# A linear-attention and two-expert-layer kernel: unit 1 directly behind unit 0, two tiles before unit 2, and another order in the first experts and at the pass ends

## The reference, cut

```python
# attention: B, H, S, D = 4, 8, 768, 48, all float32
mag = sqrt(a_re**2 + a_im**2); scale = minimum(mag, 0.999) / (mag + 1e-6)
for t in range(S):
    S_re, S_im = ar*S_re - ai*S_im + outer(k[t], v[t]), ar*S_im + ai*S_re
    y[t] = q[t] @ S_re
# first layer: x (3072 x 384), w_in (384 x 2048), w_out (2048 x 384)
h = x @ w_in
g = where(h >= 1, h, where(h <= -1, 0, (h + 1)**2 / 4))
x = g @ w_out
# second layer: 8 experts, w1 (384 x 1024), w2 (1024 x 384) each
P = exp(logits - max); 8 times: rows of P to 1, columns of P to 1, P *= N / E
out = sum over e of P[:, e] * (maximum(x @ w1[e], 0) @ w2[e])
```

## Time and profile before

| | |
|---|---|
| runs, us | 2284.01, 2279.48, 2281.38 (median 2281.38) |
| profiled execution | 2283.22 us, its span 2281.4 us |
| TensorE busy | 2235.4 us (98%) |
| VectorE, ScalarE, GpSimd busy | 76%, 44%, 21% |
| mean granted TensorE clock | 0.994 of 2.4 GHz |
| instructions | 38084 |

### The profile page before, as it was taken

One profiled execution on the slowest core, in us unless ns is written; L12 is line 12 of the kernel. 1 busy time (PEld: TensorE's weight loads), 2 busy tenths in 40 slices (PEclk: granted clock), 3 DMA queues, 4 the chain that ended last, 5 costly groups with the idle time before them and its releaser, 6 DMA issues. The chain is left out here.

```text
span 2281.4 us, 38084 instructions
## 1 busy us (share of the span) xinstructions
PE 2235.4 (98%) x13741; PEld 2081.1 (91%) x13741; DVE 1728.4 (76%) x3042; ACT 1012.3 (44%) x1716; POOL 467.8 (21%) x310
## 2 busy tenths in 40 slices
PE   5899999999999999999999999999999999999999
PEld 4799999999999889999998999999998999999998
DVE  7788888888855877776778777777777777777775
ACT  6566666566555433344334433344333433334332
POOL 0000000000000423232223322233222322233222
PEclk9899999999999999999999999999999999999999
DMA  5111111111103031111110231111110211101111
GB/s 169 39 52 53 50 50 50 50 50 50 43 29 139 28 111 56 35 49 56 55 56 28 83 111 56 46 37 55 55 55 28 84 56 56 54 30 56 55 56 28
DMA packets 70726, 131.34 MB, mean 58 GB/s; under 512 B 5512, under 2 KB 36488, under 8 KB 70536
## 3 DMA queue, kind: packets, MB, share of 16 engines
q1 hardware_dynamic: 70536, 129.14, 17.4%
HBM read 114.96 MB, written 14.16 MB: 57 GB/s over the span
## 5 line engine op out<-in xcount | busy, mean ns | idle before, releaser
L606 POOL TENSOR_TENSOR h_l<-u_s,h_h 128x512 fp32r<-128x512 f32 x192 | 246.4, 1304 | 1601.5 <-ACT h_h L863 1601.5
L1777 PE MATMUL bank<-w_h,h_h 128*128 128x384 f32 x1536 | 515.7, 336 | 5.0 <-POOL h_l L606 3.8
L1779 PE MATMUL bank<-w_h,h_l 128*128 128x384 f32 x1536 | 514.8, 335 | 0.0
L1778 PE MATMUL bank<-w_l,h_h 128*128 128x384 f32 x1536 | 514.6, 335 | 0.0
L1584 PE MATMUL bank<-x_l,w_h 128*128 128x512 f32 x1056 | 414.6, 393 | 0.0
L1583 PE MATMUL bank<-x_h,w_h 128*128 128x512 f32 x1056 | 414.4, 392 | 0.0
L1585 PE MATMUL bank<-x_h,w_l 128*128 128x512 f32 x1056 | 413.5, 392 | 0.0
L1381 DVE SCALAR_TENSOR_TENSOR acc<-bank,prob,acc 128x384 f32<-128x384 f32 x352 | 214.6, 613 | 183.7 <-PE bank L1779 181.0
L1777 PEld LDWEIGHTS bank<-w_h,h_h 128*128 128x128 f32 x1536 | 289.1, 188 | 9.0 <-POOL h_l L606 5.4
L1778 PEld LDWEIGHTS bank<-w_l,h_h 128*128 128x128 f32 x1536 | 289.0, 188 | 2.0
L852 ACT ACTIVATE p_s<-bank 128x512 f32<-128x512 f32 x96 | 57.4, 598 | 523.2 <-PE bank L1585 522.9
(11 more groups left out here) (188 smaller groups left out, 3999.1 us busy)
## 6 DMA issues: line engine op xcount, KB each, us to landing
stage<-w_ SPq DMA_DIRECT2D x48, 768.0 KB, 6.6
w_raw<-w_ SPq DMA_DIRECT2D x96, 384.0 KB, 3.6
qb<-q_in_ SPq DMA_DIRECT2D x24, 192.0 KB
kb<-k_in_ SPq DMA_DIRECT2D x24, 192.0 KB
vb<-v_in_ SPq DMA_DIRECT2D x24, 192.0 KB
x_hi<-x2h_s SPq DMA_DIRECT2D x36, 128.0 KB, 1.8
x_lo<-x2l_s SPq DMA_DIRECT2D x36, 128.0 KB, 1.8
x_h<-x_hi SPq DMA_DIRECT2D x3, 1536.0 KB, 11.3
```

What stands on the lines that cost most here:

```text
L606: pool.tensor_tensor(tiles_of(h_l, name), group_sum(name), tiles_of(h_h, name).bitcast(F32), ALU.subtract).then_inc(hl_done, 1)
L1777: pe.matmul(dst, h_h[:, f, t_], w2h[:, fw], start=n == 0, stop=False)
L1778: pe.matmul(dst, h_h[:, f, t_], w2l[:, fw], start=False, stop=False)
L1779: mm = pe.matmul(dst, h_l[:, f, t_], w2h[:, fw], start=False, stop=n == 3)
```

## The change

On TensorE units 0 and 1 have a sequence of their own (`first_units`), in which p and r of unit 1 follow x of unit 0, one weight piece goes between r and the products of q and k, and `mm_in(0)`, `mm_in(1)`, `mm_out(0)` follow unit 1. ScalarE and VectorE get matching orders. Units 2 and 3 take tiles from tables. Eight pieces go ahead of the first p, with high parts one more ahead, and twelve pieces' low parts are TensorE's, four VectorE's. `scale_factor` is cut in two, and scale_sum(1) goes between its halves. In group 1 of the experts, `w1_sums` goes ahead of sum 11, `w1_hi` behind the high part of 21_0, and two parts of `w1_lo` ahead of the low part of 22_1; `sink_rows(5)` is no longer cut. Steps 4 and 5 of `xt_sums` go into the loop over y.

```diff
-        LEAD, BY_PE = 7, 13
-        SPLIT_AT = [LEAD + 2, LEAD + 2, LEAD + 4, BY_PE, BY_PE + 1, BY_PE + 2, BY_PE + 3, BY_PE + 3, BY_PE + 3]
+        LEAD, BY_PE = 8, 12
+        SPLIT_AT = {2: ((BY_PE, BY_PE + 2), (BY_PE + 2, BY_PE + 3)), 3: ((BY_PE + 3, 2 * TILES), (0, 0))}
+        def tile_of(u, s_):
+            return {2: (2, None, 3, 4), 3: (5, None, 6, 7)}[u][s_] if u < 4 else 4 * (u - 2) + s_
+        def tile_before(u, s_):
+            return {2: (1, 2, None, 3), 3: (4, 5, None, 6)}[u][s_] if u < 4 else 4 * (u - 2) + s_ - 1
+        def out_of(u, s_):
+            return {2: (None, 1, 2, 3), 3: (None, 4, 5, None)}[u][s_] if u < 4 else 4 * (u - 2) + s_ - 2
...
@@ GpSimd, group @@
                 for name in LOW:
+                    if one and name == "22_1":
+                        w1_lo(g + 1, 1 - j, range(2))
                     h_lo(g, name)
...
-                        w1_lo(g + 1, 1 - j)
+                        w1_lo(g + 1, 1 - j, range(2, 3) if one else range(3))
...
@@ ScalarE @@
+            def first_unit():
+                stacks(0, 0)
+                stacks(0, 1)
+                p_sq(1)
+                p_root(1)
+                first_lo(LEAD + 1, LEAD + 2)
+                scale_sq(3)
+                y_out(0)
+                x_hi(0)
+                scale_root(3)
+                first_hi(LEAD + 3, BY_PE)
+            def second_unit():
+                first_lo(LEAD + 2, LEAD + 3)
+                stacks(1, 0)
+                stacks(1, 1)
+                first_lo(LEAD + 3, BY_PE)
+                scale_sq(4)
+                y_out(1)
+                x_hi(1)
+                g_sq(0)
+                g_hi(0)
+                g_sq(1)
+                p_sq(2)
+                p_root(2)
+                scale_root(4)
...
-            first_hi(0, 1)
+            first_hi(0, 2)
             for i in range(LEAD):
-                first_hi(i + 1, i + 2)
+                first_hi(i + 2, i + 3)
                 first_lo(i, i + 1)
-            first_hi(LEAD + 1, LEAD + 2)
+            first_hi(LEAD + 2, LEAD + 3)
...
                 h_hi(g, "21_0")
+                if one:
+                    for part in range(3):
+                        w1_hi(ex + j, g + 1, 1 - j, part)
...
@@ VectorE, first_unit and second_unit @@
                 scale_sum(3)
-                scale(3)
                 state_add(0)
                 x_lo(0)
...
                 by_k(1)
-                blocks(1, 1, 5)
+                scale(3)
+                blocks(1, 1, 2)
                 masked(1)
-                blocks(1, 5, NI)
+                blocks(1, 2, NI)
+                state_add(1)
                 scan_init(1)
-                scan(1, 0, 2)
-                state_add(1)
-                scan(1, 2, 3)
                 x_lo(1)
+                scan(1, 0, 3)
+                g_max(0)
                 scan(1, 3, 4)
+                g_lo(0)
                 final(2)
...
-            FIRST_LO = {2: ((), (), (), (BY_PE, BY_PE + 1)), 3: ((), (BY_PE + 1, BY_PE + 2), (), ()),
-                        4: ((BY_PE + 2, BY_PE + 3), (), (), ())}
+            FIRST_LO = {2: ((), (), (BY_PE, BY_PE + 2), ()), 3: ((), (), (BY_PE + 2, BY_PE + 3), ()),
+                        4: ((BY_PE + 3, BY_PE + 4), (), (), ())}
...
             scale_sum(0)
+            scale_first(0)
+            scale_sum(1)
             scale_factor(0)
-            scale_sum(1)
             scale_by(0)
...
@@ VectorE, group @@
                 if second:
                     sink_columns(3)
+                    w1_sums(ex + j, g + 1, 1 - j)
...
-                next_x2(4)
+                if j:
+                    next_x2(4)
...
-                next_x2(5)
...
-                if second:
-                    sink_rows(5, (0,))
                 for k in range(PB):
                     if second and k == 2:
-                        sink_rows(5, (1,))
-                    if k == (2 if second else 0) and (nxt or j == 0):
+                        sink_rows(5)
+                    if not second and k == 0 and (nxt or j == 0):
                         w1_sums(ex + j, g + 1, 1 - j)
+                    if j == 0 and k in (5, 6):
+                        next_x2(k - 1)
...
@@ TensorE @@
+            def first_units():
+                first_lo(0, LEAD)
+                p_by_tokens(0)
+                first_lo(LEAD, LEAD + 1)
+                r_by_tokens(0)
+                q_and_k(0)
+                scores(0)
+                first_lo(LEAD + 1, LEAD + 2)
+                y_sum(0)
+                state_sum(0)
+                x_by_channels(0)
+                p_by_tokens(1)
+                r_by_tokens(1)
+                first_lo(LEAD + 2, LEAD + 3)
+                q_and_k(1)
+                scores(1)
+                first_lo(LEAD + 3, BY_PE)
+                y_sum(1)
+                state_sum(1)
+                x_by_channels(1)
+                mm_in(0)
+                mm_in(1)
+                mm_out(0)
...
+            for u in range(2, UNITS):
                 p_by_tokens(u)
+                tile_in(tile_of(u, 0))
                 r_by_tokens(u)
+                tile_out(out_of(u, 0))
                 q_and_k(u)
+                tile_in(tile_of(u, 1))
+                tile_out(out_of(u, 1))
                 scores(u)
+                tile_in(tile_of(u, 2))
+                tile_out(out_of(u, 2))
                 y_sum(u)
                 state_sum(u)
+                tile_in(tile_of(u, 3))
                 x_by_channels(u)
+                tile_out(out_of(u, 3))
```

More of the change, by code:

```diff
@@ L593, in w2_lo, with w1_lo @@
                                        ALU.subtract).then_inc(w2_low, 1)
-            def w1_lo(g, j):
+            def w1_lo(g, j, parts=range(3)):
                 raw_ = quad(j)
                 h, l, to = w1s[j]
-                for part, (w, r_) in enumerate(((slice(W_11, W_22), raw_[:, :, :, 0]),
-                                                (slice(W_22, S_1), raw_[:, 1:3, :, 1]),
-                                                (slice(S_1, NW), to[:, S_1:NW]))):
+                for part in parts:
+                    w, r_ = ((slice(W_11, W_22), raw_[:, :, :, 0]), (slice(W_22, S_1), raw_[:, 1:3, :, 1]),
+                             (slice(S_1, NW), to[:, S_1:NW]))[part]
                     pool.wait_ge(w1_high, g * 3 + part + 1)
@@ L610, in group @@
                 g = ex * QUADS + j
+                one = isinstance(g, int) and g == 1
                 for name in LOW:
+                    if one and name == "22_1":
+                        w1_lo(g + 1, 1 - j, range(2))
                     h_lo(g, name)
@@ L745, in unit @@
                     p_sq(u + 1)
-                tile_hi(t)
-                tile_sq(t + 1)
+                tile_hi(tile_before(u, 1))
+                tile_sq(tile_of(u, 1))
                 if even and u >= 4:
@@ L801, in _ @@
             scale_root(2)
-            for u in range(UNITS):
+            first_unit()
+            second_unit()
+            for u in range(2, UNITS):
                 unit(u)
@@ L874, in group @@
                 g = ex * QUADS + j
-                zero = isinstance(g, int) and g == 0
+                zero, one = (isinstance(g, int) and g == i for i in range(2))
                 keep_p1(g, 0)
@@ L903, in group @@
                 elif nxt or j == 0:
-                    for part in range(3):
-                        w1_hi(ex + j, g + 1, 1 - j, part)
+                    if not one:
+                        for part in range(3):
+                            w1_hi(ex + j, g + 1, 1 - j, part)
                     w2_hi(ex + j, g + 1, 1 - j)
@@ L932, in scale, with scale_first @@
             def scale(u):
+                scale_first(u)
                 scale_factor(u)
                 scale_by(u)
-            def scale_factor(u):
+            def scale_first(u):
                 n = 4 * u
@@ L943, in scale_factor @@
                 dve.scalar_tensor_tensor(yr_u[:], sq[:, 1], 3.0, yr_u[:], ALU.subtract, ALU.mult).then_inc(scaling, 1)
+            def scale_factor(u):
+                n = 4 * u
+                sq, yr_u = sq_(u), yr_(u)
                 dve.wait_ge(scaling, n + 2)
```

109 lines of the change are left out of this document (38 added, 71 removed).

## The result

The changed kernel takes **2270.68 us** (median of 5 runs, 2269.91 to 2271.69) against 2281.52 for the kernel before (median of 5, 2279.48 to 2284.01). The ratio is 0.9955, with a 95% interval of 0.9944 to 0.9966. The profiled execution took 2270.68 us itself, span 2268.8; the one of before took 2283.22, which is 1.7 above its median. So the two traces differ by 12.5 us, of which 10.8 is the change as the medians have it. Either way the change is worth half a per cent: small, but clear of the spread of the runs.

The account below looks back on a forecast made before the run. TensorE, busy 98% of the span, was taken to bound the kernel. Attention 5.5, group 1 1 and pass ends 4.5 sum to 11.0 us off, 2270.4 by the median (forecast 2270.5), range 2265 to 2277.5.

Parts of the forecast that it names:

- the attention's 5.5: Whole attention stage, steps 1 to 6 together: 5.5 us gained, range 3 to 8.
- Before the first p: Start of unit 0: first p 0.85 us sooner; eighth weight piece counted 0, up to 0.5 lost if ScalarE is late.
- r(1) at 49.5: Unit 0 to 1: TensorE starts r of unit 1 at 49.5, not 54.76, without x_lo(0)'s wait; gain so far 5.2 us.
- Tile 0 at 65.8: Unit 1: VectorE's path of 16.2 us from r lets tile 0 start at 65.8, 10.2 us sooner.
- mm_out(0) at 72.4, p(2) and r(2) at 75.6 and 79.5: Tiles 0 and 1 ahead of unit 2's p: its r starts 5.2 us sooner, with more work behind it.
- B: Rival: tile 0 gets in the way through half clock and VectorE at g_max; attention 1.5 to 2, 2274 us, chance 0.22.
- VectorE becomes the bound, r(4) at 131.6: Units 2 and 3: VectorE bounds; r of unit 4 7.8 us sooner, 6.8 after a 1 us wait for x2_lo.
- The clock, 1.3: Attention after unit 0: half-speed stretches of 3.4 us cost 1.3 us, bounds 0 and 3.4.
- Group 1, +1: Experts' group 1: 4.3 us of waits less 2.0 for late w1_sums and 1.3 beside GpSimd gains 1 us.
- Pass ends, 4.5: Ends of passes 0 and 1: 3.1 us of h_l waits and 1.4 of low clock saved, 4.5 (2.5 to 4.8).
- C: Rival: VectorE bounds to unit 5 and late weights, then GpSimd, hold up group 1; 2278.4 us, chance 0.12.
- D: Rival: slower, as the clock does not recover from gaps between 66 and 127 us; 2286 us, chance 0.04.

Follow-up runs that it names:

- x1: Kernel before with only the change's new pass ends (next_x2(4) and next_x2(5) moved later); 2275.78 us, ratio 0.9978.
- x2: Changed kernel with group 1 of the experts back in its old order; 2269.78 us.
- x3: Changed kernel with only scale_sum(1) put back behind scale_factor(0) on VectorE; 2270.89 us.
- s1: Changed kernel with scale_sum(1) back behind scale_factor(0) and ScalarE's high parts one piece less ahead; 2272.48 us.
- z1: Kernel before with only scale(3) moved behind by_k(1) on VectorE and its root behind x_hi(0) on ScalarE; 2275.83 us, ratio 0.9974.
- z2: Kernel before with scale(3) and its root moved later, plus the new pass ends; 2269.77 us, ratio 0.9952.
- x9: Changed kernel with scale(3) back ahead of unit 0's state on VectorE and its root ahead of y_out(0) on ScalarE; 2276.14 us.
- x5: Changed kernel with the tiles of units 2 and 3 back where they were before; 2268.64 us.
- b1: Changed kernel with the tiles of units 2 and 3 back and group 1's w1_sums and their high part late again; 2266.25 us, ratio 0.9934.
- x7: Changed kernel with group 1's w1_sums and their high part back behind the sums of 22 and 11; 2267.25 us.

## Why the prediction was right, and where it was not

The median came out at 2270.7 where 2270.5 was forecast. That close, it is partly luck. In the two traces the attention gives 9.3 us for the 5.5 that were said, group 1 -0.7 for +1, and the pass ends 4.0 for 4.5. The medians can be split too, since x1 has the new pass ends alone and x2 those and the new attention: 5.4 for the pass ends, 6.0 for the attention (2275.78 - 2269.78) and -0.9 for group 1 (x2 against the changed kernel), each uncertain by 2 us or more. So the attention's 5.5 was right for the typical execution, and the miss in group 1 is made up by small excesses elsewhere.

The attention's 5.5 is itself a difference of two errors. The working of the new schedule was some 4 us too late: 0.5 at r(1), 1.1 from there to tile 0, 1.6 from r(2) to r(4) and 1.0 for a wait that never came (steps 2, 3 and 5). The profiled execution of before, from which it was subtracted, was late as well: its r(4) is 4.4 us behind that of x1, with the same code.

1) *Before the first p*: 0.85 us said, 0.94 measured at p(0) (29.19, was 30.13). But little of it reached r(0) in x3 (0.2), since ScalarE stands between. The eighth piece was put at 0, "up to 0.5 if ScalarE is late": ScalarE is what decides there, and without the high parts' move it costs 2.0 (s1).

2) *r(1) at 49.5*: 48.96. This is the term that matters. z1 shows it alone, 4.9 us by the medians, and z2 against x1 gives 6.0; x9 has it from the other side, with the longer wait for the scores in it. The prediction had its mechanism in full, the wait of x_lo(0) here and the late scores in step 3.

3) *Tile 0 at 65.8*: 64.21. The stretch from r(1) took 15.25 us where 16.3 was said, by VectorE's path as the step had it (the first part, r to the two kt, takes 2.5 and not 3.1). z1's tile 0 comes at 68.91 only, and its r(4) is no later. So the gain of this step over z1's was given back behind tile 0; the prediction counted part of it on.

4) *mm_out(0) at 72.4, p(2) and r(2) at 75.6 and 79.5*: 70.80, 74.38 and 77.99, each some 1.2 to 1.6 sooner, as tile 0 was; from tile 0 to r(2) it took 13.8 us, and 13.7 was said. g_max(0)'s wait stood where the prediction had put it, 1.33 us in front of final(2). That the whole move is worth less than nothing (x5: 2.0 us by the medians, b1 against x7: 1.0) was one half of B, VectorE at g_max(0) in front of p, at a price far smaller than B's.

5) *VectorE becomes the bound, r(4) at 131.6*: right in kind (27.47 of 28.72 us). r(4) came at 129.84. From r(2) it took 51.85 us, the 1.4 of the low stretch at 126.9 included, where 52.1 was said without one, so this step was 1.6 us too long. The wait of 1 us for x2_lo never came. One of the same size for the x of unit 3 did, at the first tile of the next group, inside the stretch:

```profile
126.30 0.39 PE L1626 MATMUL bank<-xh,w_in_h 128*128 128x256 f32 x1 [1.07 <-DVE xl L1130]
```

6) *The clock, 1.3*: the amount held, the place did not. The changed kernel's low stretch at 72.3, in front of p(2) and r(2) as the step had it, costs nothing: from tile 0 to r(2) it took 13.78 us, and x9, with no low stretch there, took 13.79. The one at 126.9 costs 1.4 (x5, above). So a low stretch did not cost the same everywhere. Of before's 15.3 us low, the 6.8 at 53.0 go with scale(3)'s waits: the three kernels with scale(3) in its old place (before, x1, x9) all have a stretch of 6.8 us that starts at 51 to 53, and in the other eleven none starts between 40 and 68. The rest does not go with it: x9 has no other between r(1) and r(4).

7) *Group 1, +1*: -0.7 in the pair of traces, +0.7 if the five executions of the old order (mean 50.2) are set against the six of the new with w1_sums early (mean 49.45), and -0.9 by the medians (x2), with overlapping runs. So no gain is shown, and x7 shows 2.5 us lost by w1_sums and their high part alone. The working was right in its main part. The weights landed late:

```profile
767.95 1.35 DVE L1322 TENSOR_TENSOR w_raw<-stage 128x256 f32<-128x256 f32 x1 [1.37 <-PE bank L1628]
769.22 0.41 DVE L1323 TENSOR_TENSOR w_raw<-stage 128x256 f32<-128x256 f32 x1
...
766.46 2.55 POOL L617 TENSOR_TENSOR h_l<-u_s,h_h 128x512 fp32r<-128x512 f32 x2 [9.31 <-ACT h_h L895]
...
780.24 0.44 PE L1831 MATMUL bank<-w_h,h_h 128*128 128x384 f32 x1 [1.52 <-POOL h_l L617]
781.61 0.44 PE L1831 MATMUL bank<-w_h,h_h 128*128 128x384 f32 x1 [0.57 <-POOL h_l L617]
```

The page names TensorE as what ended the 1.37 us, but its product was long there. The weights' issue at 761.03 with 6.8 us to landing gives 767.8, and w1_sums starts at 767.95. The 2.1 us of waits for h_l are the "2.0 of 2.5" of the working. x7 keeps the other moves and is 2.5 better in group 1, 46.83 against 49.1 to 49.4 where no low stretch lies in either.

8) *Pass ends, 4.5*: 4.0 or 4.1 behind the last column sum in every pair. The h_l waits are 1.4 in four, where 0.7 was said; the other 1.6 or so is the low stretch that followed one of them, which none of the new kernels has.

The rule of the Trainium skill that step 7 weighed ("SBUF — State Buffer", "Who interferes with whom") fares as follows. The first sum of w1 is recorded from 767.95 to 769.30, inside which GpSimd's h_l pair ends at 766.46 + 2.55 = 769.01; the sum takes 1.35 us where the second, of the same shape, takes 0.41. The trace agrees with the exclusion, then: the instruction ends 0.3 us after GpSimd's. It cost 0.9 us (1.35 - 0.41), where 1.3 was worked out for C; VectorE started 1.1 us before GpSimd's pair ended, and was done sooner behind it than its own 0.41. The step that the prediction compared, 1.30 us against 0.18, is a weaker witness, since it has one SBUF input and the sentence is on two.

That C, B and D did not happen can be read in the same places: r(4) at 129.84, the clock at 0.90 or more, no group-1 wait above 1.52.

What stays open: why the low stretches fall where they do. In the changed kernel those at 72.3 and 782.3 us follow waits of 2.2 and of 1.5 and 0.6 us. But x2 and the changed kernel, the same up to group 1, differ in them (3.4 against 6.4 us from r(1) to r(4)), after the same waits: the changed kernel and x3 have one at 126.5 to 126.9, and the five others with these tiles have none. No run was made on that.

## What to carry to other kernels

Cut each trace at a few marks that all versions share, and compare stretch by stretch; a gain that reaches the last mark of its stage is a gain, one that fills a wait before it may only move work. Where two engines are both near full, look for the one operation that makes the chain wait, here the scale for unit 3 in front of the next unit's input: moving it gave half of this change, because it left a chain of waits and landed in a wait of the same engine. Tiles put into TensorE's gaps gave nothing. One profiled execution of a kernel with many short waits is a sample: compare its own time with the median before taking a difference of traces as the change's, and where one edit is taken out of a change, look whether the others still fit without it.

## What was not expected of the hardware

- The code up to r(4) being the same, it took 84.63 us from r(1) in one execution (before) and 81.24 in another (x1), with 15.3 and 10.9 us at the lower clock. That fewer waits of TensorE make a kernel steadier is not shown: x9, which has scale(3)'s waits, spans 2.3 us in 11 runs, and z1, which has not, 6.5 in 12 (before 8.8 in 21, changed 1.8 in 5).
- A stretch at the lower clock can be free. From r(0) to r(1) the changed kernel took 15.07 us with one (34.7) in it, and x2, x3 and x5 took 15.07 with none.
- What excludes VectorE and GpSimd from each other shows as a longer instruction and not as idle time. In the changed kernel a product of the normalisation that takes 0.36 us elsewhere took 1.61 and ended at 787.68, 0.2 us after GpSimd's pair:

```profile
786.07 1.61 DVE L1440 TENSOR_TENSOR prob<-prob,tot 128x192 f32<-128x192 f32 x1
...
783.85 3.62 POOL L603 TENSOR_TENSOR w_l<-w_raw,w_h 128x768 fp32r<-128x768 f32 x2
```
